# Lead of a fused attention and feed-forward kernel: group sums and first mean on TensorE, first tile's steps two slots later, sums of v at other slots

## What is computed

```python
# attention: q, k, v are (4, 8, 576, 64), f32; factor = 4, scale = 1/8
q_d, k_d, v_d = means of q, k, v over groups of 4 positions          # (4, 8, 144, 64)
out_d = softmax(scale * q_d @ k_d.T) @ v_d                           # coarse attention
out_up = np.repeat(out_d, 4, axis=2)
scores = np.where(abs(i - j) < 4, scale * q @ k.T, -1e9)             # local attention
x = out_up + softmax(scores) @ v                                     # -> (4, 576, 512)
# first feed-forward part
xn = (x - mean(x)) / sqrt(var(x) + 1e-6) * g_ln
x = x + relu(xn @ w_ch1) @ w_ch2                                     # w_ch1 512x2048, w_ch2 2048x512
# second part, x_prev is x shifted by one position
xk = mu_k * x + (1 - mu_k) * x_prev ;  xr = mu_r * x + (1 - mu_r) * x_prev
out = sigmoid(xr @ w_r) * (relu(xk @ w_k) ** 2 @ w_v)                # w_k 512x1024, w_v 1024x512
```

## Time and profile before

| | before |
|---|---|
| median of three runs | 840.8 us (840.16 to 841.81) |
| the profiled execution | 841.76 us |
| its span | 839.8 us |
| PE busy | 796.0 us (95%) |
| DVE, ACT, POOL busy | 452.7, 289.4, 261.4 us |
| granted TensorE clock, mean | 0.971 |

### The profile page before, as it was taken

How to read it: one execution, slowest core, us unless ns; L and a number is a source line. 1 busy time by engine, 2 the same in 40 slices (tenths; PEclk the granted TensorE clock), 3 DMA queues, 4 the chain that set the end, 5 groups by cost and what they waited for, 6 DMA issues and landing times.

```text
span 839.8 us, 14450 instructions
## 1 busy us (share of the span) xinstructions
PE 796.0 (95%) x5820; PEld 724.5 (86%) x5820; DVE 452.7 (54%) x745; ACT 289.4 (34%) x657; POOL 261.4 (31%) x274
## 2 busy tenths in 40 slices
PE   4779995999999999999999999999999999999998
PEld 4668894999999899999899999999788888888886
DVE  5468553533654434564454352255768667575664
ACT  5554431323322422332322232155533433333322
POOL 4446544523425432432542341200311111111111
PEclk9579997999999999999999999999999999999999
DMA  9781143021044102023100000361202002001010
GB/s 171 193 239 62 34 78 90 2 46 43 1 82 77 44 21 40 30 50 81 57 12 21 29 2 11 104 225 52 79 1 72 29 1 76 0 1 51 1 50 26
DMA packets 113058, 47.94 MB, mean 57 GB/s; under 512 B 92768, under 2 KB 101984, under 8 KB 112992
## 3 DMA queue, kind: packets, MB, share of 16 engines
q1 hardware_dynamic: 112992, 47.02, 22.1%
HBM read 37.57 MB, written 9.44 MB: 56 GB/s over the span
## 4 chain that ended last, share of the span: by engine, by line
PE 79%; DVE 4%; SPq 4%; POOL 4%; issue 3%; ACT 3%; DMA 2%; POOLq 0%; DVEq 0%; ACTq 0%
PE psY L911 20%; PE psH L894 20%; PE psY L964 11%; PE psH L945 11%; PE psA L927 6%; SPq L487 4%; PE psA L802 2%; DMA v_raw<-in_v_dram 2%; PE psA L829 2%; PE psA L815 1%; PE psA L784 1%; PE psA L770 1%; PE psA L757 1%; POOL x L683 1%; POOL v_raw L632 1%
## 5 line engine op out<-in xcount | busy, mean ns | idle before, releaser
L1473 DVE SCALAR_TENSOR_TENSOR h_lo<-psH,h_hi 128x288 fp32r<-128x288 f32 x128 | 58.1, 454 | 213.2 <-ACT h_hi L1226 213.0
L911 PE MATMUL psY<-h_hi,w_hi 128*128 128x288 f32 x512 | 161.7, 316 | 11.3 <-DVE y_tmp L1389 11.2
L894 PE MATMUL psH<-xc_hi,w_hi 128*128 128x288 f32 x512 | 157.4, 307 | 2.4 <-DVE xc_lo L1361 2.4
L894 PE MATMUL psH<-xc_hi,w_lo 128*128 128x288 f32 x512 | 152.7, 298 | 0.0
L911 PE MATMUL psY<-h_hi,w_lo 128*128 128x288 f32 x512 | 151.9, 297 | 0.0
L911 PE MATMUL psY<-h_lo,w_hi 128*128 128x288 f32 x512 | 151.9, 297 | 0.0
L894 PE MATMUL psH<-xc_lo,w_hi 128*128 128x288 f32 x512 | 151.7, 296 | 0.0
L1226 ACT ACTIVATE h_hi<-psH 128x288 fp32r<-128x288 f32 x128 | 52.5, 410 | 234.1 <-PE psH L894 234.0
L731 POOL TENSOR_TENSOR relu_k<-relu_k 128x512 f32<-128x512 f32 (+1 forms) x40 | 38.7, 967 | 252.4 <-ACT relu_k L1187 252.4
L911 PEld LDWEIGHTS psY<-h_hi,w_hi 128*128 128x128 f32 x512 | 97.1, 190 | 19.0 <-DVE y_tmp L1389 12.0
L894 PEld LDWEIGHTS psH<-xc_hi,w_hi 128*128 128x128 f32 x512 | 98.0, 191 | 4.8 <-issue 2.7
(11 more groups left out here) (170 smaller groups left out, 1450.7 us busy)
## 6 DMA issues: line engine op xcount, KB each, us to landing
w_raw<-in_moe_w_ch_dram SPq DMA_DIRECT2D x8, 1024.0 KB, 8.4
x_scratch<-x SPq DMA_DIRECT2D x8, 576.0 KB, 3.3
out_dram<-gate SPq DMA_DIRECT2D x18, 256.0 KB, 2.1
raw<-in_q_dram SPq DMA_DIRECT2D x112, 36.0 KB, 1.9
raw<-in_k_dram SPq DMA_DIRECT2D x96, 36.0 KB, 2.0
v_raw<-in_v_dram SPq DMA_DIRECT2D x12, 288.0 KB
x_sh<-x_scratch SPq DMA_DIRECT2D x3, 1026.0 KB, 5.8
v_win<-in_v_dram SPq DMA_DIRECT2D x14, 208.0 KB
```

The source lines that it names most:

```text
L894: ins = mm(psH[:, m % 2, 0:N], ws[a][:, kt, f * P:(f + 1) * P], xx[bb][:, kt], start=(kt == 0 and i == 0), stop=(kt == KT - 1 and i == 2))
L911: ins = mm(psY[:, d, 0:N], ws[a][:, f, d * P:(d + 1) * P], hs[bb][:, m % 2], start=(f == 0 and i == 0), stop=(f == NF1 - 1 and i == 2))
L1473: nc.vector.scalar_tensor_tensor(out=h_lo[:, m % 2], in0=psH[:, m % 2, 0:N], scalar=0.0, in1=h_hi[:, m % 2].bitcast(F32), op0=ALU.max, op1 ...
```

## The change

The group sums of k and q in the lead come from TensorE: a matrix `groups` (96x24, ones where row p belongs to group g) is multiplied by k and q as loaded, 36 matmuls of one 96x128 block each, into one pair of banks, and DVE copies the results out in four copies. The mean of tile 0 is 12 matmuls of ones by x, without POOL. The coarse exponentials come ahead of the third window's; DVE takes over the coarse normalisation, the third window's, and the copies of the coarse transposes. Tile 1's attention steps stand two slots later, as do V and R of tile 0. In tile 0 DVE's `attend(2m)` comes ahead of the weight pieces, which are one m later. The flips of tile 2 and the sums of v get other slots, and SP's first loads another order.

```diff
-             ("S", 0, 2, 3), ("Tk", 0, 2, 0), ("Sd", 0, 0, 2), ("Sd", 0, 1, 1), ("PT", 0, 0, 3), ("AV", 0, 0, 3),
...
+    FIRST = [("Tk", 0, 0, 0), ("Tq", 0, 0, 1), ("S", 0, 0, 2), ("Tk", 0, 1, 0), ("Tq", 0, 1, 1), ("S", 0, 1, 0),
+             ("S", 0, 2, 1), ("Tk", 0, 2, 2), ("G", 0, 0, 3), ("Sd", 0, 0, 0), ("Sd", 0, 1, 2), ("PT", 0, 0, 1),
+             ("AV", 0, 0, 3), ("PT", 0, 1, 0), ("PdT", 0, 0, 1), ("PdT", 0, 1, 2), ("OD", 0, 0, 1), ("OD", 0, 1, 2),
+             ("AV", 0, 1, 0), ("PT", 0, 2, 1), ("AV", 0, 2, 2), ("M", 0, 0, 3)]
...
-    OWN_FIRST = [(1, "V", 0), (8, "R", 0)]
+    OWN_FIRST = [(2, "V", 0), (10, "R", 0)]
+    BEHIND = 2
...
+        later += [(SLOTS * (u - 1) + s + (BEHIND if u == 1 else 0), kind, u, n) for s, kind, n in LATER]
...
-    FLIPS_THIRD = [(-11, "k", 0, 0), (-9, "k", 0, 1), (-6, "k", 1, 0), (-5, "k", 1, 1), (-4, "q", 0, 0), (-2, "q", 0, 1)]
+    FLIPS_THIRD = [(-12, "k", 0, 0), (-10, "k", 0, 1), (-8, "k", 1, 0), (-4, "k", 1, 1), (-3, "q", 0, 0), (-2, "q", 0, 1)]
...
-        for g, (s, before) in enumerate(((28, 3), (30, 1), (35, 4), (39, 3))):
+        behind = BEHIND if b == 1 else 0
+        for g, (s, load) in enumerate(((14 + behind, 8), (20 + behind, 15 + behind), (27 + behind, 21 + behind), (39, 31))):
             V_SUM[SLOTS * (2 * b - 2) + s] = (b, g)
-            V_LOAD[SLOTS * (2 * b - 2) + s - before] = (b, g)
+            V_LOAD[SLOTS * (2 * b - 2) + load] = (b, g)
-    W1_M = {0: [(1, 0), (1, 1)], 1: [(1, 2), (1, 3)], 2: [(2, 0)], 3: [(2, 1)], 4: [(2, 2)], 5: [(2, 3)],
-            6: [(3, 0)], 7: [(3, 1)], 8: [(3, 2)], 9: [(3, 3)]}
+    W1_M = {0: [(1, 0), (1, 1)], 1: [(1, 2)], 2: [(1, 3)], 3: [(2, 0)], 4: [(2, 1)], 5: [(2, 2)],
+            6: [(2, 3)], 7: [(3, 0)], 8: [(3, 1)], 9: [(3, 2)], 10: [(3, 3)]}
@@ sync @@
             load_window(2)
+            load_w1(0)
...
-            load_w1(0)
             load_w2(0)
+            load_later(0)
             load_w1(1)
-            for j in range(RAW):
-                load_later(j)
+            load_later(1)
             load_window(3)
+            load_w1(2)
             load_window(4)
-            load_w1(2)
             load_w1(3)
+            load_later(2)
@@ gpsimd, lead @@
             norm(0, 1)
-            norm(0, 2)
-            norm_d(0, 0)
-            norm_d(0, 1)
             v_sum(0, 3)
-            for n in range(NW_U):
-                x_sum(0, n)
@@ tensor @@
+            def group(what, n):
+                for x, c in enumerate(TURN[what][n]):
+                    src = turn_source(what, n, x)
+                    bank, at = group_place(what, c)
+                    for j in range(KT):
+                        ins = mm(pairs[pair_at(place_of["G", 0, 0])][:, bank, at + j * GW:at + (j + 1) * GW], src[:, j * P:(j + 1) * P],
+                                 groups[0:W, :], start=True, stop=True, skip_group_check=True)
+                ins.then_inc(grouped, 1)
...
+                    if u == 0:
+                        pe.wait_ge(x_made, n + 1)
+                        for j in range(KT):
+                            ins = mm(pairs[pair_at(i)][:, 0, at], ones[:], x[:, 0, j, at], start=(j == 0), stop=(j == KT - 1),
+                                     skip_group_check=True)
+                        continue
...
             turn("Tk", 1)
+            group("Tk", 0)
             turn("Tq", 1)
+            group("Tq", 0)
             scores(0, 1)
             scores(0, 2)
+            group("Tk", 1)
+            group("Tq", 1)
             turn("Tk", 2)
+            group("Tk", 2)
             scores_d(0, 0)
             scores_d(0, 1)
             turn_p(0, 0)
             values(0, 0)
             turn_p(0, 1)
-            values(0, 1)
-            turn_p(0, 2)
             turn_d(0, 0)
             turn_d(0, 1)
             values_d(0, 0)
             values_d(0, 1)
+            values(0, 1)
+            turn_p(0, 2)
             values(0, 2)
@@ scalar, lead @@
             pt_o(0, 0)
+            exp_d(0, 0)
+            exp_d(0, 1)
             exp_first(2)
-            exp_d(0, 0)
             pt_o(0, 1)
...
@@ vector @@
+            def sums_first():
+                dve.wait_ge(grouped, N_TURN0)
+                banks = pairs[pair_at(place_of["G", 0, 0])]
+                for what, dst, c0, nc_ in (("Tk", kdT, 0, NW_U), ("Tk", kdT, NW_U, NW_U), ("Tq", qdT, 0, 2), ("Tq", qdT, 2, 1)):
+                    bank, at = group_place(what, c0)
+                    src = banks[:, bank, at:at + nc_ * KT * GW].rearrange("p (c j g) -> p c j g", j=KT, g=GW)
+                    ins = nc.vector.tensor_copy(dst[:, :, c0 * GW:(c0 + nc_) * GW].rearrange("p j (c g) -> p c j g", g=GW), src)
+                ins.then_inc(summed, 1)
...
-            sum_first("Tk", 0)
-            sum_first("Tq", 0)
             mask(0, 0)
-            sum_first("Tk", 1)
-            sum_first("Tq", 1)
             mask(0, 1)
             sum_of_p(0, 0)
+            sums_first()
             mask(0, 2)
-            sum_first("Tk", 2)
             top_of_d(0, 0)
+            top_of_d(0, 1)
             sum_of_p(0, 1)
-            top_of_d(0, 1)
+            sum_of_d(0, 0)
+            norm_d_first(0)
+            sum_of_d(0, 1)
+            norm_d_first(1)
+            pdt_first(0)
+            pdt_first(1)
             sum_of_p(0, 2)
+            norm_first(2)
...
+                attend(2 * m)
                 if u == 0:
                     for x_ in W1_M.get(f, []):
                         lo_weight("w1", *x_)
-                attend(2 * m)
```

More of the change, by code:

```diff
@@ L78, in fused_kernel @@
     for u in range(1, NU):
-        later += [(SLOTS * (u - 1) + s, kind, u, n) for s, kind, n in LATER]
+        later += [(SLOTS * (u - 1) + s + (BEHIND if u == 1 else 0), kind, u, n) for s, kind, n in LATER]
     for u in range(NU):
@@ L190, in fused_kernel @@
         ident = sb(ctx, "ident", [P, P])
+        groups = sb(ctx, "groups", [P, GW])
         ones = sb(ctx, "ones", [P, P])
@@ L265, in fused_kernel @@
         turned = sem("turned")
+        grouped = sem("grouped")
         turn_out = sem("turn_out")
@@ L364, in wait_step_out @@
                 eng.wait_ge(turn_out, turn_of[kind, u, n] + 1)
+            elif kind == "G":
+                eng.wait_ge(summed, 1)
             elif kind == "Sd":
@@ L411, in turned_place @@
         def turned_place(kind, u, n):
-            i = {("PT", 1): 1, ("PT", 2): 2, ("PdT", 1): 1}.get((kind, n), 0) if u == 0 else 0
+            i = {("PT", 1): 1, ("PdT", 1): 2}.get((kind, n), 0) if u == 0 else 0
             return probT if i == 0 else probT_first[:, i - 1]
@@ L419, in turn_source, with group_place @@
             return (k_first if what == "Tk" else q_first)[0:W, TURN[what][n][x]]
+        def group_place(what, c):
+            if what == "Tk":
+                return c // NW_U, c % NW_U * KT * GW
+            return c // 2, (NW_U + c % 2) * KT * GW
         def vw_slot(w):
@@ L615, in _ @@
                                     pattern=[[-1, P]], channel_multiplier=1).then_inc(consts, 1)
+            chain(nc.gpsimd.memset(groups[:], 1.0))
+            chain(nc.gpsimd.affine_select(out=groups[:], in_=groups[:], compare_op=ALU.is_ge, fill=0.0, base=0,
+                                          pattern=[[-FACTOR, GW]], channel_multiplier=1))
+            nc.gpsimd.affine_select(out=groups[:], in_=groups[:], compare_op=ALU.is_ge, fill=0.0, base=REACH,
+                                    pattern=[[FACTOR, GW]], channel_multiplier=-1).then_inc(consts, 1)
             nc.gpsimd.memset(ones[:], 1.0).then_inc(consts, 1)
@@ L882, in up_b @@
                 u, f = divmod(m, NF1)
-                if u == 0 and f % 4 == 0:
+                if u == 0 and f % 4 == 0 and f:
                     pe.wait_ge(w_split, lo_index["w1", f // 4, KT - 1] + 1)
@@ L890, in up_b @@
                 for kt in range(KT):
+                    if m == 0:
+                        pe.wait_ge(w_split, lo_index["w1", 0, kt] + 1)
                     if f == 0 and kt % 2 == 0:
@@ L1078, in pt_o @@
                     act.wait_ge(av_done, w)
+                elif n == 2:
+                    act.wait_ge(od_done, 1)
                 copy(turned_place("PT", u, n)[0:kn].rearrange("p (a c) -> p a c", a=2), pairs[pair_at(i)][0:kn, :, 0:KT * W]).then_inc(pt_out, 1)
@@ L1204, in _ @@
             pt_o(0, 0)
+            exp_d(0, 0)
+            exp_d(0, 1)
             exp_first(2)
-            exp_d(0, 0)
             pt_o(0, 1)
-            exp_d(0, 1)
-            pt_o(0, 2)
-            pdt_o(0, 0)
-            hi_weight("w1", 0, 0)
-            pdt_o(0, 1)
-            hi_weight("w1", 0, 1)
-            hi_weight("w1", 0, 2)
             od_o(0, 0)
             od_o(0, 1)
-            hi_weight("w1", 0, 3)
+            hi_weight("w1", 0, 0)
+            pt_o(0, 2)
+            for kt in range(1, KT):
+                hi_weight("w1", 0, kt)
             hi_x(0)
@@ L1440, in sigmoid @@
                 chain(nc.vector.reciprocal(g, g))
```

(24 more changed lines are left out.)

34 lines of the change are left out of this document (22 added, 12 removed), and 2 rows, old and new, of the table FIRST.

## The result

The kernel after takes 830.71 us, median of four runs (829.2 to 832.35), against 841.3 us (840.16 to 844.0) for four runs of the kernel before: a ratio of 0.987, 95% interval 0.9837 to 0.9903. The prediction was 829.0 us.

A forecast was written before the change was run, and what follows sets the result against it. PE was taken as the bound nearly everywhere, so only its waits or half clock could give time back. 841.76 + 10.2 - 12.4 - 4.5 - 0.75 - 3.0 - 1.3 = 830.0, less 0.96 is 829.0 us; range 814 to 837.

The forecast's parts named there:

- lead, `up_b(0)`: Start of the kernel: up_b(0) at 56.0 us, 10.2 us later than before, with group instructions at 0.20 us.
- long wait at tile 1: Respaced sums of v remove PE's 10.22 us y_tmp wait, 0.65 ahead of Sd and 1.55 of half clock: 12.4 us.
- starts of tiles 3 and 5: Sums of v ahead of add_y cost 1.0 us and twice 1.7 us there; 4.5 us taken off.
- tile 0: V's wait, order, clock: V's wait covered, 0.75 us; attend(2m) ahead of weight pieces, 3.0 of 3.9; clock opening earlier, 1.3 of 2.7.
- second piece of w_ch2: SP's weight loads after the lead, wanted by the fourth block: near, but nothing, or 1 us against.
- The mean: End of the lead: 24 instructions with 128-column weights on TensorE, 4.8 us at 0.20 each.
- The choice of 0.20 by the size of the weights: Lead: 0.20 us to a group instruction, within bounds 0.10 and 0.25, as weights of the same size stand nearest.
- cheap groups: Rival in the lead: group and mean instructions cost 0.10 us, total 817.4; chance 0.32 together with a mixture.
- The fourth sum: Sum of v at slot 39: load behind three raw loads, about 13 us; its user is OD of tile 2, slot 42.

The follow-up runs named there:

- the sums alone: Kernel before with the new slots of the sums of v and nothing else: 825.01 us, ratio 0.9819.
- the early piece: Changed kernel with the whole old lead, and the second piece of w_ch2 loaded ahead of the last raw loads: 818.41 us, ratio 0.9719.
- the unused tile: Changed kernel with the whole old lead and one unused tile of 96 bytes a partition behind ident: 819.25 us, ratio 0.9735.
- the weight pieces first: Changed kernel with old lead and early second piece of w_ch2, DVE's weight pieces ahead of attend(2m) again: 824.76 us, ratio 0.9809.

## Why the prediction was right

The total was right, 829.0 against 830.71 us. Term by term, as differences of spans:

| step | predicted | measured |
|---|---|---|
| lead, `up_b(0)` | +10.2 | +13.1 |
| long wait at tile 1 | -12.4 | -12.6 |
| starts of tiles 3 and 5 | -4.5 | -6.8 |
| tile 0: V's wait, order, clock | -0.75 - 3.0 - 1.3 = -5.05 | -4.8 |
| second piece of w_ch2 | nothing, or 1 | 1.5, within the row above |
| second part | none | +1.8 |

The sum was better than its terms, and that is luck: the lead was 2.9 us too cheap and the starts of tiles 3 and 5 were 2.3 us too small, which cancel, and what is left is mostly the second part, which no term had.

*The lead* fell short by 2.9 us, in three places. (The prediction's terms up to the last group add to 30.6 and not 30.8, and those behind it to 0.2 less than its 56.0 needs, so by its own terms it fell short by 3.3.) The groups were forecast to end at 30.8 and the coarse scores to start at 32.3; with 0.208 us to an instruction instead of 0.20 these were 31.7 and 33.0, 0.7 us. From there to the mean I had 16.3 us along ACT's exponentials; it was 18.0. PE has only 2.6 us of waits there (0.89, 0.34, 0.43 and 0.89), so the transposes and products themselves, at half clock, were the chain. The mean took 5.4 us and not 5.0, at 0.225 us an instruction: it has 96 moving columns, as the rows from which I read 0.21 to 0.25, and I had priced it at 0.20 all the same. The choice of 0.20 by the size of the weights held for the groups. For a load of P columns the Trainium skill (TensorE: Matmul & The Clock Gate, LDWEIGHTS) gives P / 1.2 ns and names no clock, 107 ns for these; that it holds at any clock was the prediction's reading. The rows at full clock agree, 0.11 us from one 128-column load with its matmul to the next. The trace of the new lead does not: there it is 208 ns, and the measurement decides. If the load by that rule set the pace, the groups would have been an estimated 7.3 us cheaper (72 x 0.101). The rival "cheap groups" needed an open clock or that quick load, and had neither.

*The long wait.* The size was right, and the run with the sums alone confirms the cause. What the prediction had wrong is that it was the sole cause: in the kernel after, with its flips, delay and lead, the old sums bring back only 6 of 12.6 us. There the load stands behind 16 raw DMAs and not 24.

*Tiles 3 and 5.* I added up the waits that the view of waits shows. The stretches from V to V were 3.4 us each over the 65.5 us of the undisturbed tiles, and comparing them would have given 6.8 us ahead of the result. That was in the trace of before. The largest piece that the waits leave out is a half clock: behind the second wait of 1.72 us, at the start of tile 5, the matmuls stand 0.24 us apart from 408.71 to 411.83, which costs 1.6 us. A matmul of that stretch, and the stretch in the columns of the earlier trace rows, with a recorded clock of 0.57:

```profile
408.71 0.44 PE L911 MATMUL psY<-h_lo,w_hi 128*128 128x288 f32 x1
```
```profile
408.00:412.00 4.00, 4.00 (x23) 3.81 (x20) 1.57 (x5) 1.55 (x8) 1.15 (x1) 0.57 0.26 73
```

The prediction counted that price at tile 1 and not here. Behind the same wait at the start of tile 3 (274.91) the clock stayed up.

*Tile 0.* The first two blocks with V took 8.0 us before (45.80 to the next step at 53.78) and take 5.2 now (58.88 to 64.12): 2.7 us for V's wait and the clock, where I had 2.05; V itself at full clock was the part left out. The rest of the row is 2.1 us, and with the 1.5 us that the piece of w_ch2 cost, the order gave 3.6, where I had 3.0 of 3.9 seen. Taken back by itself it costs 6.3 us, more than the waits that one sees before: the wait for x is 3.0 us, as with the respaced sums alone in the old order, and not 1.3 as before, and a half clock of 1.6 us stands behind it. The delay by two slots is worth 1.3 to 3.1 us, 0.75 of it V's wait.

*The fourth sum* was covered, as forecast: its load leaves SP at 136.11 and POOL sums at 145.88 without a wait.

*The second piece of w_ch2* cost 1.5 us, beyond the 1 us that I had as its dear end.

*The second part.* That a 96-byte tile ahead of the other buffers would move the matmuls of the second part by 1.5% was in no step. It makes 1.5 of the 1.8 us. Beside it, the first eighth of the second part takes 1.5 us more in some executions, in kernels with and without the tile. It does not explain the two groups of run times of the kernel after (829.2, 829.6 and 831.8, 832.4): the profiled execution, 832.35 us, is of the slower group and has none of it. What does is open.

*The version to keep* is neither kernel: everything of the change but its lead, 817.14 us, or 818.41 with the early piece. Both beat the kernel after by 12 to 14 us and the one before by 2.8%.

## What to carry to other kernels

Measure each tile from one recurring step to the next and compare with the shortest: what an undisturbed tile takes, and what the others lose, comes out whole, where the view of waits shows only a part and leaves out a half clock behind a wait. Work moved to the engine that bounds the span has to be priced at the clock that stretch really has; here 72 small matmuls of 15 us in sum took 2.2 us off a wait. And a bundle of edits should be run part by part even where it is faster: this one held a loss of 13 us under a gain of 24.

## What the runs showed of the hardware

- The recorded clock of the new lead is 1.00 between 5 and 40 us, while eight transposes take 1.5 us as at a recorded 0.50 and not 0.88; with the unused tile the 136 instructions between 20 and 40 us take the same 15.48 us at a recorded 1.00 as at 0.50 before. The record can miss a half clock; known durations show it.
- Group matmuls, transposes and scores with PE busy 14.37 of 15 us left the durations at those of 1.2 GHz, as did the mean's 24 instructions at 51.01. Behind fourteen fp32r matmuls of 288 columns the transposes at 4.70 took the time of 2.4 GHz.
- In the kernel after the first matmuls of `up_b(0)` stand 0.13 us apart (full clock), from 59.96 to 63.08 us 0.24 apart, and then 0.13 again. The clock fell for 3 us in the midst of dense work; the idle 2.44 us lie ahead of all of it. Each of the mean's 24 instructions, up to 56.4, still has the duration of half clock, so the clock rose behind the last of them.
- A wait in the midst of dense work can cost more than itself. Behind waits of 1.72 us (before, tile 5) and 3.0 us (the sums alone; the weight pieces first) 3.1 us at half clock follow, 1.6 us lost; behind the same 1.72 us in tile 3 none does.
- An unused tile of 96 bytes to a partition made 480 matmuls of the second part slower, 0.2089 us from start to start against 0.2057; with the matrix in a tile of 128 bytes they took 0.2077.
